# Local attention values: two of seven offsets as scaled copies on ScalarE

## What is computed

```
# q, k, v: (4, 8, 576, 64)
q_d, k_d, v_d = means over 4 neighbouring tokens        # 144 pooled tokens
out_up    = repeat(softmax(scale * q_d @ k_d.T) @ v_d, 4)
mask      = |i - j| < 4                                 # 7 offsets
out_local = softmax(where(mask, scale * q @ k.T, -1e9)) @ v
x   = (out_up + out_local) as (2304, 512)
y   = ((x @ w_a) * (x @ w_b)) @ w_out                   # 512 -> 1536 -> 512
h   = y @ w_in;  solu = h * softmax(h)                  # 512 -> 1024
out = layer_norm(solu) * g_ln @ w_out2                  # 1024 -> 512
```

## Time and profile before

| | us |
|---|---|
| median of three runs | 837.2 (833.18 to 838.5) |
| the profiled execution, device time | 840.08 |
| its span, first to last instruction | 838.3 |
| PE busy | 783.5 (93%) |
| DVE busy | 586.1 (70%) |
| ACT busy | 249.8 (30%) |
| POOL busy | 185.9 (22%) |

### The profile page before, as it was taken

One profiled execution on the slowest core, in us unless ns is written; L12 is line 12 of the kernel. 1 busy time (PEld: TensorE's weight loads), 2 busy tenths in 40 slices (PEclk: granted clock), 3 DMA queues, 4 the chain that ended last, 5 costly groups with the idle time before them and its releaser, 6 DMA issues. The chain is left out here.

```text
span 838.3 us, 11870 instructions
## 1 busy us (share of the span) xinstructions
PE 783.5 (93%) x4392; PEld 715.3 (85%) x4392; DVE 586.1 (70%) x1012; ACT 249.8 (30%) x583; POOL 185.9 (22%) x143
## 2 busy tenths in 40 slices
PE   5769899799799979999989999999999999999997
PEld 5648889789799979989989999999887888888885
DVE  2579899979879896879688697212346766676663
ACT  4453434233133322133213222224412222222221
POOL 3455555308404230002000323121200000000000
PEclk9999999999899998999999999999999999999999
DMA  9999968465767674767555553356111011111110
GB/s 186 220 217 209 245 176 223 138 203 162 229 194 239 229 197 138 192 171 158 137 178 170 170 160 104 113 182 221 51 51 50 26 51 51 51 32 44 51 39 25
DMA packets 94682, 119.11 MB, mean 142 GB/s; under 512 B 17057, under 2 KB 56739, under 8 KB 94625
## 3 DMA queue, kind: packets, MB, share of 16 engines
q1 hardware_dynamic: 79904, 108.85, 46.4%
q10 hardware_dynamic: 14721, 9.51, 4.1%
HBM read 97.49 MB, written 20.84 MB: 141 GB/s over the span
## 5 line engine op out<-in xcount | busy, mean ns | idle before, releaser
L826 PE MATMUL psum<-x_hi,w_hi 128*128 128x384 f32 x576 | 201.5, 350 | 5.5 <-DVE x_lo L1321 5.4
L827 PE MATMUL psum<-x_lo,w_hi 128*128 128x384 f32 x576 | 195.7, 340 | 0.0
L828 PE MATMUL psum<-x_hi,w_lo 128*128 128x384 f32 x576 | 195.5, 339 | 0.0
L826 PEld LDWEIGHTS psum<-x_hi,w_hi 128*128 128x128 f32 x576 | 110.6, 192 | 10.5 <-issue 9.9
L827 PEld LDWEIGHTS psum<-x_lo,w_hi 128*128 128x128 f32 x576 | 110.6, 192 | 0.0
L828 PEld LDWEIGHTS psum<-x_hi,w_lo 128*128 128x128 f32 x576 | 110.4, 192 | 0.0
L1327 DVE TENSOR_TENSOR ab_f<-psum,a_sb 128x384 f32<-128x384 f32 x72 | 39.9, 554 | 99.8 <-PE psum L828 63.3
L826 PE MATMUL psum<-ab_hi,wo_hi 128*128 128x384 f32 x288 | 101.7, 353 | 3.6 <-issue 3.6
L828 PE MATMUL psum<-ab_hi,wo_lo 128*128 128x384 f32 x288 | 98.6, 343 | 0.0
L827 PE MATMUL psum<-ab_lo,wo_hi 128*128 128x384 f32 x288 | 98.5, 342 | 0.0
L1622 POOL TENSOR_TENSOR ab_lo<-ab_f,ab_hi 128x384 fp32r<-128x384 f32 x24 | 37.4, 1557 | 187.6 <-ACT ab_hi L1102 187.6
(11 more groups left out here) (139 smaller groups left out, 1300.2 us busy)
## 6 DMA issues: line engine op xcount, KB each, us to landing
wo_hi<-wo_hi_scratch SPq DMA_DIRECT2D x54, 256.0 KB, 2.7
wo_lo<-wo_lo_scratch SPq DMA_DIRECT2D x54, 256.0 KB, 3.1
k_u<-in_k SPq DMA_DIRECT2D x11, 576.0 KB
v_u<-in_v SPq DMA_DIRECT2D x11, 576.0 KB
k_u<-in_k SPq DMA_DIRECT2D x17, 288.0 KB
v_u<-in_v SPq DMA_DIRECT2D x17, 288.0 KB
raw<-in_v SPq DMA_DIRECT2D x8, 576.0 KB, 7.0
raw<-in_q SPq DMA_DIRECT2D x8, 576.0 KB, 9.2
```

The source lines that it names most:

```text
L826: mm(dst, wh, xh, start=first, stop=False, skip_group_check=not check)
L827: mm(dst, wh, xl, start=False, stop=False, skip_group_check=not check)
L828: last = mm(dst, wl, xh, start=False, stop=end, skip_group_check=not check)
```

## The change

In each of the ten units, the products of offsets 0 and 1 move to ScalarE. A new ScalarE function `unit_values` runs at steps 11 to 14 (positions 6 to 9 for a first unit from tile 1 on). Each step issues six ACTIVATE copies of 128x64 with a per-partition scale, so 24 for a unit: offset 0 into `acc`, offset 1 into `tmp[:, 1]`. VectorE makes offsets 2 to 6 in steps 10 to 14, sums them in `tmp[:, 0]` with four additions, adds the two ScalarE products at step 15 and joins the sums at step 16. `accT` serves as a third buffer for products, so the wait for the transposition of the unit before moves from END to step 12. ScalarE waits for the scaled probabilities (`u_normed`), for `v_u` and for `acc` to be free; VectorE waits at step 15 for ScalarE (`u_act_values`), and gives `v_u` back there.

```diff
+ACT_VALUES, ACT_SUM = 11, 15
...
+            def unit_values(u, step):
+
+                e, half = divmod(step - ACT_VALUES, 2)
+                if step == ACT_VALUES:
+                    act.wait_ge(s.u_normed, u - 1)
+                    act.wait_ge(s.v_loaded, 16 * loads_to(u, PAD, WT))
+                    at_least(act, s.acc_ready, u - 2)
+                dst = acc[:, :, :] if e == 0 else tmp[:, 1]
+                for h in (2 * half, 2 * half + 1):
+                    for t in range(TPP):
+                        i = h * TPP + t
+                        last = A(dst[:, h, t * D:(t + 1) * D], v_u[:, h, (e + t) * D:(e + t + 1) * D], ACT.Copy,
+                                 scale=p_u[:, e, i:i + 1])
+                if half == 1:
+                    last.then_inc(s.u_act_values, 1)
...
                     if step == 9:
                         unit_exp(2 * (m + 1) + half)
+                    if ACT_VALUES <= step < ACT_SUM:
+                        unit_values(2 * (m + 1) + half, step)
...
-                e = step - (EDGE + 3)
-                if 0 <= e < EDGE:
-                    if e == 0:
+                e = step - (EDGE + 3) + 2
+                slots = [acc[:, :, :], tmp[:, 1], tmp[:, 0], tmp[:, 2], turned_slot, tmp[:, 2], turned_slot]
+                if 2 <= e < EDGE:
+                    if e == 2:
                         dve.wait_ge(s.v_loaded, 16 * loads_to(u, PAD, WT))
-                        at_least(dve, s.acc_ready, u - 2)
+                    if e == 4:
+                        at_least(dve, s.x_turned, 2 * (u - 2))
...
-                for i in range(e, e + (2 if e == EDGE - 1 else 1)):
-                    if i < 2 or step == END:
-                        continue
-                    local.wait(max(marks[EDGE + i - 1], used[-1]))
-                    if i == EDGE:
-                        dve.sem_inc(s.v_used, 1)
-                    last = V.tensor_tensor(acc[:, :, :], acc[:, :, :], tmp[:, (i - 1) % 3], ALU.add)
+                if 4 <= e <= EDGE:
+
+                    local.wait(max(marks[EDGE + e - 3], used[-1]))
+                    last = V.tensor_tensor(tmp[:, 0], tmp[:, 0], slots[e - 1], ALU.add)
+                    used.append(local.mark(last))
+                if step == ACT_SUM:
+
+                    dve.wait_ge(s.u_act_values, 2 * (u - 1))
+                    dve.sem_inc(s.v_used, 1)
+                    last = V.tensor_tensor(acc[:, :, :], acc[:, :, :], tmp[:, 1], ALU.add)
+                    used.append(local.mark(last))
+                if step == STEPS - 1:
+                    local.wait(used[-1])
+                    last = V.tensor_tensor(acc[:, :, :], acc[:, :, :], tmp[:, 0], ALU.add)
                     used.append(local.mark(last))
```

More of the change, by code:

```diff
@@ L365, in build_program @@
         p_turned pT_out out_mm_d out_d_ready
-        loc_chain k_used v_used q_used u_sub_ready u_exped acc_ready x_turned x_hi_ready x_lo_ready
+        loc_chain k_used v_used q_used u_sub_ready u_exped u_normed u_act_values acc_ready x_turned x_hi_ready x_lo_ready
         w_hi_ready w_lo_by_vector w_lo_by_pool wo_hi_ready wo_lo_by_vector wo_lo_by_pool
@@ L1345, in _ @@
             heads3 = [128, 4, TPP, D]
+            turned_slot = accT[:, :, :].rearrange("p t n -> p (t n)").rearrange("p (h x) -> p h x", h=4)
             def local_step(m, g, step, marks, used):
@@ L1385, in local_step @@
                     local.link(V.reciprocal(u_inv[:, :], u_den[:, :]))
-                    local.link(V.tensor_tensor(p_u[:, :, :], p_u[:, :, :],
-                                               u_inv[:, :].unsqueeze(1).to_broadcast([128, EDGE, 4 * TPP]), ALU.mult))
-                e = step - (EDGE + 3)
-                if 0 <= e < EDGE:
-                    if e == 0:
-                        dve.wait_ge(s.v_loaded, 16 * loads_to(u, PAD, WT))
-                        at_least(dve, s.acc_ready, u - 2)
[L1393 to L1396, removed]
+                    V.tensor_tensor(p_u[:, :, :], p_u[:, :, :],
+                                    u_inv[:, :].unsqueeze(1).to_broadcast([128, EDGE, 4 * TPP]), ALU.mult
+                                    ).then_inc(s.u_normed, 1)
+                    dve.wait_ge(s.u_normed, u - 1)
+                e = step - (EDGE + 3) + 2
+                slots = [acc[:, :, :], tmp[:, 1], tmp[:, 0], tmp[:, 2], turned_slot, tmp[:, 2], turned_slot]
+                if 2 <= e < EDGE:
+                    if e == 2:
+                        dve.wait_ge(s.v_loaded, 16 * loads_to(u, PAD, WT))
+                    if e == 4:
+                        at_least(dve, s.x_turned, 2 * (u - 2))
+                    if e > 4:
+                        local.wait(used[EDGE + e - 5])
+                    last = V.tensor_tensor(slots[e].rearrange("p h (t d) -> p h t d", d=D),
                                            v_u[:, :, e * D:e * D + TPP * D].rearrange("p h (t d) -> p h t d", d=D),
@@ L1412, in local_step @@
                     dve.wait_ge(s.xup_loaded, 16 * (u - 1))
-                    at_least(dve, s.x_turned, 2 * (u - 2))
                     V.tensor_tensor(accT[:, :, :].rearrange("p t (h d) -> p h t d", d=D),
```

## The result

The changed kernel takes 832.5 us in the median of 11 runs (828.97 to 836.96), the kernel before 837.93 beside it (11 runs). The ratio is 0.9939, with an interval of 0.9911 to 0.9967: 5.1 us less, and surely less, though under the 1% that I called the limit of a plain verdict. 833.0 was forecast. The profiled execution took 832.51 us against 840.08 before, 7.6 us less.

The account below looks back on a forecast made before the run. TensorE, busy 93%, was taken as the bound, so sparing VectorE counts only where TensorE waits for it. Tiles 0, 1 and 4 give 2.2, 1.2 and 0.8, together 4.2 us: 837.2 - 4.2 = 833.0, range 828 to 840.

Parts of the forecast that it names:

- The sum: Over the whole kernel: 2.2 us from tile 0, 1.2 from tile 1 and 0.8 from tile 4, together 4.2 us less.
- ScalarE's price: Scaled copies on ScalarE: 0.21 us each, 1.3 us per step of six, 50 us in all, judged from two `out_d` copies.
- The cover of the copies: ScalarE's copies are hidden in its idle time ahead of `ab_hi` and `a_sb`, except in tile 0 at positions 9 and 10.
- The late gate in tile 0: Twelve copies ahead of `a_sb` bring the gate that stood at 104.39 1.3 us later, carried to the end of tile 0.
- Tile 0's 2.2 us: Two units spare VectorE 1.75 us each, the late gate loses 1.3: 2.2 us gained at the END at 163.26.
- every microsecond that it is spared is passed on: Tile 0, 104 to 171 us: VectorE, busy 65.94 of 67 us, passes all spared time to its next gate, rest and END.
- Tile 1's 1.2 us: VectorE is spared 1.75 us, but END cannot pass the landing of `xup` at 218.6: 219.82 - 218.6 = 1.2 us gained.
- new waits of VectorE: VectorE's waits at step 15 for ScalarE's copies in tiles 1 and 4: nothing; without idle cover, up to 1 us a tile.
- more, by the clock: Rival, chance 0.18: shorter stalls in tiles 1 and 0 spare drops of TensorE's clock, 5.2 us on top: 828.
- Tiles 2 and 3: No gain in either: END is bound by `xup` in tile 2 and by ScalarE's exponential in tile 3.
- Nothing: Rival, chance 0.20: copies cost 0.31 us each or tile 1's gate is late too, leaving 836 to 839.
- slower: Rival, chance 0.12: ScalarE becomes the one waited for, deciding at 2.4 us per six copies; at 0.5 us a copy, 843 to 847.

## Why the prediction held, and where it did not

**The sum.** 4.2 us were forecast and 5.1 (2.8 to 7.5) measured. Putting the products back gives all of it back, so its origin, two products less at step 16, is shown. The way from there to the time was not the forecast one: 4.2 us of shorter waits were added up, and in the profiles TensorE's waits are 0.3 us shorter and the time at the lower clock makes the difference. That the sum met the result is in good part luck.

**ScalarE's price.** I took 0.21 us a copy. It is 0.24, with 335 ns for one:

```profile
L1087 ACT ACTIVATE acc<-v_u,p_u x120: 299/335/351, 100.1 to 508.8; 128x64 f32<-128x64 f32 x120
```

The Trainium skill's figures (ScalarE: Activation LUTs, "What ACT_TABLE_LOAD costs") make 332 ns and 0.24 us, an estimate from the page, and the trace agrees with them rather than with the neighbour that I chose, the `out_d` copies.

**The cover of the copies.** Of the two signs of being wrong that concern ScalarE, one did not come: VectorE waits for no copy of `acc` or `tmp`. The other did, in part. `a_sb` ends eight waits of the gate, 14.7 us in all, where it was three and 6.1 us before:

```profile
DVE ab_f L1347 <- ACT a_sb L1115: 14.7, 8, 3.3
```

With the copies of one position put behind `a_sb`, the waits are back at 5.7 us, and the median is lower by more than tile 0's share. So "at nothing" behind tile 0 was probably too good.

**The late gate in tile 0.** Forecast 1.3 us late, measured 1.04. The timeline of ScalarE against the earlier trace rows, and the gate against the earlier trace rows:

```profile
100.14 1.55 ACT L1087 ACTIVATE acc<-v_u,p_u 128x64 f32<-128x64 f32 x6 [1.35 <-issue]
101.59 1.05 ACT L1094 ACTIVATE w_hi<-w_raw 128x1024 fp32r<-128x1024 f32 x1
102.54 1.19 ACT L1016 ACTIVATE qdT<-psum 128x288 f32<-128x288 f32 x2
103.53 1.50 ACT L1087 ACTIVATE acc<-v_u,p_u 128x64 f32<-128x64 f32 x6
104.93 0.47 ACT L1115 ACTIVATE a_sb<-psum 128x384 f32<-128x384 f32 x1
```

```profile
105.43 0.56 DVE L1347 TENSOR_TENSOR ab_f<-psum,a_sb 128x384 f32<-128x384 f32 x1 [3.32 <-ACT a_sb L1115]
```

The working was right to 0.3 us, and one wide copy, or the copies put behind `a_sb`, takes the delay away.

**Tile 0's 2.2 us: not borne out.** The step in doubt is "every microsecond that it is spared is passed on". In the pair of profiles the last END came at 163.11, against 163.26. Between 104 and 171 us VectorE's value products and additions took 23.8 us instead of 27.0, so 3.2 were spared, about as costed. Its q by k products took 13.6 instead of 12.4 and one pooled scaling 0.9 more, and the late gate took 0.8: the same instructions, stretched beside GpSimd. From this pair alone one would conclude that the meetings with GpSimd ate what was spared. The other profiles show that it cannot carry that. What VectorE's products, additions and rests took in tile 0 above their undisturbed 0.95 and 0.55 us is 15.3 us before and 18.4 after, but 11.7 to 19.2 over all thirteen profiles; with the change in tile 0 and without it, the average is about the same, near 17. So less work on VectorE does not spare the meetings, but it does not add to them either, and the 3 us more in the changed kernel are within the scatter between executions. By that the spared time should shorten the tile. The timed runs with the change in tile 0 alone do not show it, with the reserve made there. So whether the step failed, and why, stays open.

**Tile 1's 1.2 us: the number by luck.** END moved from 219.82 to 218.57, within 0.1 us of the forecast. The step behind it failed: that `xup` lands at 218.6 and END cannot pass it. In the changed kernel `xup` was issued at 207.51 and landed 5.9 us later, at 213.4. END, 5.2 us behind that, started without a wait, straight behind VectorE's own work:

```profile
207.51 0.56 SPq L523 DMA_DIRECT2D xup<-xup_scratch  x1
...
xup<-xup_scratch SPq DMA_DIRECT2D x1, 384.0 KB, 5.9
...
217.71 0.94 DVE L1389 TENSOR_REDUCE p_u<-tmp 128x12 f32<-128x768 f32 x1
218.57 0.94 DVE L1445 TENSOR_TENSOR accT<-acc,xup 128x768 f32<-128x768 f32 x1
```

SyncE's order is the same, but its times are not: the load stands behind stores of pooled rows that GpSimd sums, and one of these sums took 6.68 us before and 2.73 after (last section). That this moved the load is read from the order, not tested. The stall went from 4.24 to 1.68 us, where about 3 were forecast. But the change brought a new stall of 2.34 us ahead of it, so TensorE's idle time in the tile fell by 1.6 us only:

```profile
198.22 2.55 POOL L1633 TENSOR_TENSOR raw<-raw 96x768 f32<-96x768 f32 x1
198.99 2.59 DVE L1430 TENSOR_TENSOR tmp<-tmp 128x768 f32<-128x768 f32 x1
...
200.84 1.59 POOL L1636 TENSOR_TENSOR raw<-raw 96x384 f32<-96x384 f32 x1
201.51 2.57 DVE L1351 TENSOR_TENSOR ab_lo<-ab_f,ab_hi 128x384 fp32r<-128x384 f32 x1
...
204.17 0.41 PE L828 MATMUL psum<-ab_hi,wo_hi 128*128 128x384 f32 x1 [2.34 <-issue]
```

I had costed the new waits of VectorE there at nothing, and they are nothing. What came instead is GpSimd beside VectorE. Most of the rest of the tile's 4.0 us is the clock: behind the stall, before the change, half the stretch at the lower level is 2.9 us, and there is none now.

**The clock.** The rival "more, by the clock" came true in this execution: the drop behind tile 1's stall (0.96 of 80 us) is gone, and with it some of the drop in tile 2 and all of that in tile 3, which explains most of the 0.8 and 1.0 us in tiles for which I had forecast none. In the twelve other profiles tile 1's stall is 3.4 us at most, and no drop lies behind it. In tile 2 the drop follows the wait for END, as told above. The sum of the forecast had no term for it. The clock is the likely reason that the two profiles differ by 7.6 us and the timed runs by 5.1. How much of the 5.1 is clock stays open. Of the timed runs only the mean clock of each is on record: 0.988 in the median over the 11 of the changed kernel, 0.982 over the 53 of the kernel before beside the experiments. Of 835 us, 0.006 is 5 us, which is a bound and not a share: a drop while TensorE waits costs nothing, and within one kernel the clock does not order the runs (828.97 us at 0.989, but 836.96 at 0.984 and 832.50 at 0.967).

**Tiles 2 and 3.** No gain from the change, as forecast. The causes named for their stalls are confirmed by their moves, `xup` in tile 2 and the exponential in tile 3; in tile 2 half the cause, a meeting of GpSimd and VectorE, was missed, though it stood in the trace of the kernel before (`ab_lo` 1.91 us and the product behind it 1.77).

**Tile 4.** The stall of 1.08 us is gone, 0.8 forecast.

**The other rivals.** "Nothing" and "slower" did not come; the second is real at twice as many copies.

## What to carry to other kernels

Ask of each stall what is late when the first late thing is repaired: the END of one tile was held by VectorE's load, of the next by a transfer behind other transfers in a queue, of the next by an order of two steps. Two moves in the order were worth twice what the moved work was. When small instructions go to an engine with 30% load, look at what stands between two of its deadlines, not at the share: here 1.4 us per set cost little and 2.6 too much. Two more. Price a stall with what it does to the clock behind it: in tile 2 that was another third of the stall or more. And do not explain a few microseconds of one stretch from one pair of profiles: the same code took 100.1 to 103.0 us, and a forecast can meet the measured total with its terms wrong.

## What the runs showed of the hardware

Some of VectorE's instructions are stretched beside a running GpSimd instruction, and some kinds never were. Of the changed kernel, min, median and max ns of a sum over one tensor, of a product of two from SBUF, of a pooled scaling (one small input from SBUF) and of the gate (one input from PSUM):

```profile
L1389 DVE TENSOR_REDUCE p_u<-tmp x70: 936/942/948, 69.0 to 494.2; 128x12 f32<-128x768 f32 x70
...
L1380 DVE TENSOR_TENSOR tmp<-q_u,k_u x70: 932/948/4208, 67.3 to 492.0; 128x768 f32<-128x768 f32 x70
...
L1291 DVE TENSOR_SCALAR pool_bias<-pool_max x20: 165/168/983, 73.0 to 498.2; 96x2 f32<-96x2 f32 x12, 128x2 f32<-128x2 f32 x8
...
L1347 DVE TENSOR_TENSOR ab_f<-psum,a_sb x72: 539/557/559, 69.9 to 598.8; 128x384 f32<-128x384 f32 x72
```

The sum and the gate keep their time, the product and the scaling do not, and not in every meeting: of 16 such q by k products that ran mostly beside a GpSimd instruction, four took their usual time. Which of the two engines pays differs. In the kernel before, a GpSimd sum of 96x384 in tile 1 took 6.68 us while six VectorE products and additions beside it took 0.95 us each; in the changed kernel the same sum took 2.73 us, and VectorE's neighbours of the sums behind it 1.65 to 2.59:

```profile
195.54 6.68 POOL L1605 TENSOR_TENSOR raw<-raw 96x384 f32<-96x384 f32 x1
```

What decides it, no run here shows.
